# The first unit's C12 moves to a bank of its own, and C21's activation goes ahead of C12's low part

## What is computed

```
kv  = einsum('bhsd,bhse->bhde', k, v)          # 4 batches, 8 heads, 576 rows, 64 wide
o   = einsum('bhsd,bhde->bhse', q, kv)
x   = o / sqrt(mean(o*o) + 1e-6) * g_norm      # then 2304 tokens x 512
h   = x @ w_in                                  # 512 x 2048
g   = max(h, 0) + alpha * min(h, 0)
x   = g @ w_out                                 # 2048 x 512
P   = exp(x @ w_gate - max), 8 rounds of row and column balancing
out = sum over 8 experts of P[:, e] * (max(x @ w1[e], 0) @ w2[e])   # 512 x 1024 x 512
```

## The kernel before

| step | engine, line | where in the run, us |
| --- | --- | --- |
| M5 of unit 0, first matmul | PE L1057 | 76.95 |
| M7, turning of x, M3 of unit 0 | PE L1057, L979, L1057 | 78.09, 79.13, 79.57 |
| M1, M2 of unit 1 | PE L1057 | 84.00, 85.12 |
| `second(0, 0)` | PE L1085 | 86.17 |
| C12: sum, activation, low part | DVE L775, L745, L748, L763 | 80.91 to 83.85 |
| C21: activation | DVE L745, L748 | 83.77 to 84.97 |

## Time and profile before

### The profile page before, as it was taken

One profiled execution on the slowest core, in us unless ns is written; L12 is line 12 of the kernel. 1 busy time (PEld: TensorE's weight loads), 2 busy tenths in 40 slices (PEclk: granted clock), 3 DMA queues, 4 the chain that ended last, 5 costly groups with the idle time before them and its releaser, 6 DMA issues.

```text
span 1987.5 us, 26236 instructions
## 1 busy us (share of the span) xinstructions
PE 1968.2 (99%) x10396; PEld 1770.3 (89%) x10396; DVE 791.5 (40%) x1379; ACT 810.7 (41%) x1400; POOL 1161.7 (58%) x867
## 2 busy tenths in 40 slices
PE   8999999999999999999999999999999999999999
PEld 7898999998888988888888889888889888888888
DVE  4655556554454332334423333233432333323333
ACT  5644444444433344334443333343443443333332
POOL 2766466464656655666655666655666556666553
PEclk9999999999999999999999999999999999999999
DMA  9422122122222222212232222222223222222221
GB/s 245 117 65 79 49 66 78 49 66 63 64 64 64 72 78 64 64 64 64 77 104 64 64 64 66 82 66 64 64 64 103 78 64 64 64 64 78 71 64 43
DMA packets 174985, 146.44 MB, mean 74 GB/s; under 512 B 9728, under 2 KB 141840, under 8 KB 174864
## 3 DMA queue, kind: packets, MB, share of 16 engines
q1 hardware_dynamic: 174144, 144.74, 24.8%
q10 hardware_dynamic: 720, 0.03, 0.0%
HBM read 140.01 MB, written 4.72 MB: 73 GB/s over the span
## 4 chain that ended last, share of the span: by engine, by line
PE 97%; DVE 1%; DMA 1%; ACT 0%; issue 0%; SPq 0%
PE ps L1087 17%; PE ps L1086 17%; PE ps L1085 16%; PE ps L1059 15%; PE ps L1057 15%; PE ps L1060 15%; DMA qkv<-in_v 1%; PE ps L965 1%; PE ps L1101 1%; PE ps L948 1%; PE ps L1093 0%; PE ps L979 0%; PE ps L933 0%; DVE acc L904 0%; SPq L351 0%
## 5 line engine op out<-in xcount | busy, mean ns | idle before, releaser
L452 POOL TENSOR_TENSOR w1l<-raw,w1h 128x768 fp32r<-128x768 f32 x120 | 223.2, 1860 | 740.7 <-PE ps L1060 740.0
L1087 PE MATMUL ps<-w2h,hh 128*128 128x512 f32 x1440 | 571.6, 397 | 0.0
L1086 PE MATMUL ps<-w2l,hh 128*128 128x512 f32 x1440 | 568.7, 395 | 0.0
L1057 PE MATMUL ps<-ring_parts,w1h 128*128 128x384 f32 x1680 | 563.2, 335 | 3.5 <-DVE hh L763 2.8
L1060 PE MATMUL ps<-ring_parts,w1l 128*128 128x384 f32 x1680 | 561.4, 334 | 0.0
L1085 PE MATMUL ps<-w2h,hh 128*128 128x512 f32 x1440 | 560.5, 389 | 0.0
L591 ACT ACTIVATE hh<-ps 128x384 fp32r<-128x384 f32 x240 | 118.4, 493 | 617.5 <-DVE ps L775 495.0
L1057 PEld LDWEIGHTS ps<-ring_parts,w1h 128*128 128x128 f32 x1680 | 315.6, 188 | 34.0 <-issue 3.8
L1059 PE MATMUL ps<-x_parts,w1h 128*128 128x384 f32 x960 | 322.8, 336 | 0.0
L1087 PEld LDWEIGHTS ps<-w2h,hh 128*128 128x128 f32 x1440 | 269.8, 187 | 57.3
L1060 PEld LDWEIGHTS ps<-ring_parts,w1l 128*128 128x128 f32 x1680 | 315.3, 188 | 0.0
(11 more groups left out here) (102 smaller groups left out, 1787.6 us busy)
## 6 DMA issues: line engine op xcount, KB each, us to landing
raw<-in_moe_w SPq DMA_DIRECT2D x384, 256.0 KB, 3.4
raw<-in_moe_w_in SPq DMA_DIRECT2D x48, 256.0 KB, 3.9
raw<-in_moe_w_out SPq DMA_DIRECT2D x48, 256.0 KB, 3.0
qkv<-in_q SPq DMA_DIRECT2D x16, 288.0 KB, 9.3
qkv<-in_k SPq DMA_DIRECT2D x16, 288.0 KB, 8.7
qkv<-in_v SPq DMA_DIRECT2D x16, 288.0 KB, 10.6
out<-acc SPq DMA_DIRECT2D x12, 192.0 KB, 2.5
out<-acc SPq DMA_DIRECT2D x12, 128.0 KB, 2.4
```

The lines of the kernel that those rows point to most:

```text
L452: nc.gpsimd.tensor_tensor(w1l[:, u % 2, B22:T1, :].rearrange("p m c -> p (m c)"), r[:, KW:4 * KW], w1h[:, u % 2, B22:T1, :].rearrange("p m ...
L1057: nc.tensor.matmul(bank, wh, xh, start=i in (M1, M2, M5) and kt == 0, stop=False, skip_group_check=True)
L1086: nc.tensor.matmul(ps[:, t, :], hi, wl, start=False, stop=False)
L1087: last = nc.tensor.matmul(ps[:, t, :], lo, wh, start=False, stop=closes_sum(u) and i == 1)
```

## The change

Three edits, all for unit 0 alone. M5, M3 and all that reads or writes C12 use bank 4 (`c12_bank`) in place of bank 7. M5 therefore no longer waits for C11's low part but for turn 13's `take_x`; M1 of unit 1 waits for `side_lo` 1 and no longer 2. Since turn 14 is turned while bank 4 is in use, its halves go to banks 0 and 1, and the tiles `second(0, t)` and turn 15 get waits for that. On VectorE C21's activation stands ahead of C12's low part.

```
 def x_bank(n, j):
-    return ps[:, 7 if n < TAIL_X else 4 + j, 0:HALF]
+    return ps[:, 7 if n < TAIL_X else j if n == TAIL_X + 1 else 4 + j, 0:HALF]
+def c12_bank(u):
+    return ps[:, 4, 0:BLK] if u == 0 else side_bank(u)
...
 # ScalarE: side_high(u, j) and the snapshot of M5
-nc.scalar.activation(m5s[:, :], side_bank(u), ACT.Copy).then_inc(snap, 1)
+nc.scalar.activation(m5s[:, :], c12_bank(u), ACT.Copy).then_inc(snap, 1)
...
 # VectorE: step(u)
     side_sum(u, C12, M3, u2s[:, :], 2)
-    side_split(u, C12)
+    if u > 0:
+        side_split(u, C12)
 take_columns(u, 6)
 if u < UNITS:
     if mlp(u):
+        if u == 0:
+            dve.wait_ge(side_act, 2)
         dve.wait_ge(m_done, PRODUCTS * u + M4 + 1)
         leaky(u, 2, C21, chain_bank(u), c21[:, :])
         if u == 0:
+            side_split(u, C12)
             norm(TAIL_X + 2)
...
 # TensorE: turn_x(n, j)
     if n > TAIL_X:
         pe.wait_ge(x_ready, 2 * (n - 1) + j + 1)
+    if n > TAIL_X + 1:
+        pe.wait_ge(side_lo, 2)
...
 # TensorE: product(u, i)
-bank = side_bank(u) if i in (M2, M5, M3) else chain_bank(u)
+bank = side_bank(u) if i == M2 else c12_bank(u) if i in (M5, M3) else chain_bank(u)
     # i == M1, u >= 1
-    pe.wait_ge(side_lo, 2 * u)
+    pe.wait_ge(side_lo, 2 * u if u > 1 else 1)
 elif i == M5:
-    pe.wait_ge(side_lo, 2 * u + 1)
+    if u == 0:
+        pe.wait_ge(x_ready, 2 * (TAIL_X + 1))
+    else:
+        pe.wait_ge(side_lo, 2 * u + 1)
...
 # TensorE: second(u, t), u == 0
     pe.wait_ge(xs_ready, TURNS - 1 if t < 2 else TURNS)
-    if t >= 4:
-        pe.wait_ge(x_ready, 2 * TURNS)
+    pe.wait_ge(x_ready, 2 * TURNS if t >= 4 else 2 * (TURNS - 1))
```

More of the change, by code:

```diff
@@ L590, in side_high @@
                     sc.wait_ge(c_done, 3 * u + (1 if j == C11 else 3))
-                nc.scalar.activation(hh[:, u % 2, 0, j, :], side_bank(u), ACT.Copy if mlp(u) else ACT.Relu)\
+                nc.scalar.activation(hh[:, u % 2, 0, j, :], side_bank(u) if j == C11 else c12_bank(u),
+                                     ACT.Copy if mlp(u) else ACT.Relu)\
                     .then_inc(side_hi, 1)
@@ L779, in side_sum @@
                 at = 0 if j == C11 else 2
-                block_sum(u, at, product, side_bank(u), add, kept, side_bank(u))
+                bank = side_bank(u) if j == C11 else c12_bank(u)
+                block_sum(u, at, product, bank, add, kept, bank)
                 if mlp(u):
                     dve.wait_ge(c_done, 3 * u + at + 1)
-                    leaky(u, (C11, C12).index(j), j, side_bank(u), side_bank(u))
+                    leaky(u, (C11, C12).index(j), j, bank, bank)
             def side_split(u, j):
                 dve.wait_ge(side_hi, 2 * u + (C11, C12).index(j) + 1)
-                low_part(u, j, side_bank(u)).then_inc(side_lo, 1)
+                low_part(u, j, side_bank(u) if j == C11 else c12_bank(u)).then_inc(side_lo, 1)
             def take_sum(u, t):
```

## The result

The changed kernel has a median of 1988.07 us (1986.13 to 1989.76, 22 runs), the kernel before, measured beside it, 1991.60 us (1988.56 to 1995.58, 22 runs). The ratio is 0.9982 with a 95% interval of 0.9976 to 0.9988: 3.5 us faster, between 2.4 and 4.8.

The account below looks back on a forecast made before the run. TensorE, busy 1968.2 of 1987.5 us, was taken as the bound; the steps shorten its timeline by 1.86 us, rounded to 1.9, taken off the three runs' median of 1992.48: 1990.6 us, range 1989.2 to 1992.4.

Parts of the forecast that it names:

- What bounds the kernel: TensorE: only its waits can be won, 2.8 us in two waits for VectorE's low part, 0.14% of the time.
- M5: Product M5 of unit 0, moved to bank 4: starts at 76.05 in place of 76.95, saving 0.90 us.
- turn 14: Turn 14's transposes on TensorE in unit 0: run at 78.20, with 0.06 us lost to VectorE's norm.
- M4: Product M4 of unit 0, needing C22's sum on VectorE: comes at 79.79, covered by 0.4 us.
- M1: Product M1 of unit 1: starts at about 80.87, with hardly any wait in place of 2.07 us.
- M2 of unit 1: Product waiting for C21's activation: starts at 83.19 in place of 85.12, behind about 1.1 us of stall.
- Does it last?: From `second(0, 0)` to the end: no later wait takes up the gain, 1.86 us carried on and rounded to 1.9.
- Both waits go wholly: Rival: M1 and M2 of unit 1 follow without a stall; gain 3.3 us, 1989.2 us; chance 0.07.
- Half: Rival: turn 14 or low weights later than read, or C12's chain no earlier: gain 0.85 us, 1991.6 us; chance 0.11.
- nothing: Rival: a later wait makes up M2's stall, or the wait moves wholly to `second(0, 0)`; 1992.5 us; chance 0.06.
- slower: Rival: `second(0, 0)` waits for C12's low part, ending after 86.05; at 1 us beyond, 1993.5 us; chance 0.04.

Follow-up runs that it names:

- the first C21 copy: Changed kernel with ScalarE copying C21's bank once into SBUF, C12's low part between VectorE's two instructions for C21: 1988.32 us, 0.9983 of before.

## Why the prediction was wrong

**What bounds the kernel.** Right: only TensorE's waits counted. The sentence that 2.8 us are the whole field was wrong: it took a wait's cost for its length, and so did the range, whose lower end is the two waits and their restarts, 3.3 us.

**M5, turn 14, M4, M1.** Right, each within 0.13 us of its place. The order of GpSimd's low weights behind ScalarE's snapshot went as argued (L456, before L452, began 7.28 us behind the first product and ended at 9.13; M1 came at 9.28 without a wait). The loss of 0.06 for turn 14 didn't come: it was 6.65, not 6.70. The load had been read as 0.15 ahead of its matmul, where the rows have 0.10 (85.02 and 85.12).

**M2 of unit 1.** Right: it is the new place of the wait, 1.03 us where I had about 1.1, ended by C21's activation. The waited start of L750 behind L753 was 0.03 (80.98 to 81.01) and the unwaited L768 started 0.08 ahead of the end of the one before it (82.22, 82.14), as computed: from C12's sum to the end of C21's activation it took 3.07 us, forecast 3.06. The Trainium skill's "VectorE: DVE Perf Modes", "The DRAIN you can't avoid", by which a semaphore costs nothing extra, would have made it 0.1 shorter. That M2 came 0.13 early is the rest: the sum 0.05 earlier, and 0.06 from VectorE's end to the matmul where 0.15 was taken.

**Does it last?** Right: 1901.45 against 1901.33 us.

**The step that failed** is the next one: "The three runs had a median of 1992.48, 3.15 above the profiled one; I take the same 1.9 off". The profiled execution had a mean clock of 1.000, as only 48 of 116 executions of that kernel have. In the other 68 the clock fell for a while somewhere, and of the kernel's five traces the two with a mean under 1.000 have it behind the very wait that the change shortens. The sum had no term for that. Its size follows from the table. Among executions at 1.000 the kernels differ by 1989.91 - 1987.93 = 1.98 us, which is the predicted term. For before, 68/116 times 1.93 (1991.84 - 1989.91) adds 1.13; for the changed kernel, 4/44 times 0.71 adds 0.06. The sum, 1.98 + 1.13 - 0.06 = 3.05 us, stands beside 3.1 between the means and 3.4 between the medians of these executions, and 3.5 in the first comparison, whose interval begins at 2.4. Not all of the 1.93 is this drop: traced, it cost about 1.6 us, and executions under 1 also hold drops in the attention; so the term is an estimate of 0.9 to 1.1 us, and with either end the sum lies inside that interval. The signs were on the table: the runs lay 3.15 us above the profiled execution, more than the effect that I forecast, and I carried that gap along as a constant.

**The base.** Of the 2.5 us between 1990.6 and 1988.07, 1.6 are the gain and 0.9 are the base: the three runs had a median of 1992.48, all 22 have 1991.60. The range allowed for 0.35 us of spread, where three runs spread by 0.67 and 22 by 7.0. With 1991.60 as the base the range would have begun at 1988.3 and still missed, by 0.2.

**The rivals.** None named the clock. "Both waits go wholly" had the number 1989.2 nearest to the measured one, for a reason that the trace refutes: M2 still waits. "Half", "nothing" and "slower" did not occur; `second(0, 0)` had no idle time. The range reached no further down than both waits' length, so it could not hold a wait that costs more than it lasts.

What stays open: at 1.000 the mean is rounded, so a short drop can hide there; what decides in a given execution whether the clock falls was not tried; and none of the 4 executions under 1 of the changed kernel was traced. They may be drops in the attention, drops behind the last matmul, or the wait of 1.03 us.

## What to carry to other kernels

A wait of a busy TensorE costs its length plus what the clock takes behind it: here a wait of 2.07 us cost about 1.6 us more when the clock fell, and behind waits of 2.02 to 2.07 us it fell in 4 of 7 traces. A wait of 1.03 us did so in 4 of 44 at most; but in the attention two traces have the drop behind 1.10 us. So see how the executions spread, and the mean clock of each, before trusting one trace; where the profiled execution lies several us from the median, find out where before forecasting. A wait that can't be removed may be shortened, or filled with matmuls that nobody reads.

## What the runs showed of the hardware

- TensorE behind a wait of 2.02 to 2.07 us: granted clock at 0.50 for about 3.4 us in some executions and 1.00 in others, at the same wait. It fell 0.2 to 0.7 us behind the restart (four traces), 0.2 us behind it after the wait of 3.14 us, and 0.4 us ahead of it in the wait of 2.67 us. In the attention it fell twice behind a wait of 1.10 us.
- 12 more matmuls in a row, put into a wait of 2.07 us, made a kernel 1.6 us faster over 22 executions.
- A VectorE instruction of 128x384 with its data in SBUF alone took 1.77 and 2.07 us beside a GpSimd subtraction, 0.62 and 0.55 us with the copy in PSUM. GpSimd's seems to be held in turn: in the first C21 copy an instruction of 128x256 (L445) took 1.06 us beside VectorE's second one on the copy, where its like takes 0.73 to 0.75.
